# Where VectorE sums a step's bonus: after the previous step's mask, or between the next step's scale and this step's mask

## What is computed

```python
for t in range(S):
    kt, vt, rt = (k[:, :, t], v[:, :, t], r[:, :, t])
    cur = np.einsum('bhd,bhe->bhde', u[None] * kt, vt)
    y[:, :, t] = np.einsum('bhd,bhde->bhe', rt, state + cur)
    state = w[None, :, :, None] * state + np.einsum('bhd,bhe->bhde', kt, vt)
```

## Time and profile before

| | |
|---|---|
| median of 3 runs | 385.12 us (384.98 to 385.4) |
| the profiled execution | 385.27 us |
| its span, first to last instruction | 383.5 us |
| mean granted TensorE clock | 1.000 of full speed |
| PE busy | 369.9 us, 96% |
| DVE busy | 235.0 us, 61% |
| ACT busy | 189.4 us, 49% |
| POOL busy | 94.5 us, 25% |

### The profile page before, as it was taken

How to read it: one execution, slowest core, us unless ns; L and a number is a source line. 1 busy time by engine, 2 the same in 40 slices (tenths; PEclk the granted TensorE clock), 3 DMA queues, 4 the chain that set the end, 5 groups by cost and what they waited for, 6 DMA issues and landing times.

```text
span 383.5 us, 9099 instructions
## 1 busy us (share of the span) xinstructions
PE 369.9 (96%) x3206; PEld 290.6 (76%) x3206; DVE 235.0 (61%) x433; ACT 189.4 (49%) x409; POOL 94.5 (25%) x110
## 2 busy tenths in 40 slices
PE   5698999999999999999999999999999999999996
PEld 5677788878777344577888888888888888888885
DVE  6978787878774301587756556555555555555550
ACT  1344554545434440676564456445644564465452
POOL 4678788878682020100000000000000000000000
PEclk9999999999999999999999999999999999999999
DMA  7899999999999999600011002000200020002002
GB/s 234 286 333 344 400 393 405 399 393 354 405 327 409 390 414 413 249 0 2 1 46 38 0 0 84 0 0 0 82 0 0 0 82 0 0 0 82 0 2 82
DMA packets 21797, 63.76 MB, mean 166 GB/s; under 512 B 3088, under 2 KB 6816, under 8 KB 21392
## 3 DMA queue, kind: packets, MB, share of 16 engines
q1 hardware_dynamic: 20864, 63.09, 43.4%
q10 hardware_dynamic: 912, 0.39, 0.5%
HBM read 58.75 MB, written 4.72 MB: 165 GB/s over the span
## 4 chain that ended last, share of the span: by engine, by line
PE 92%; DVE 2%; DMA 2%; issue 1%; ACT 1%; POOL 1%; SPq 0%; DVEq 0%; ACTq 0%
PE bank L638 11%; PE bank L637 11%; PE bank L636 11%; PE bank L378 6%; PE pair L426 6%; PE pair L636 6%; PE pair L637 6%; PE pair L638 6%; PE bank L623 4%; PE pair L414 3%; PE pair L397 3%; PE bank L585 3%; PE bank L447 3%; PE bank L565 2%; DMA vb<-v 2%; PE bank L438 2%
## 5 line engine op out<-in xcount | busy, mean ns | idle before, releaser
L926 DVE TENSOR_TENSOR gf<-bank,sg 128x512 f32<-128x512 f32 x72 | 49.8, 691 | 58.3 <-ACT sg L1133 58.0
L1133 ACT ACTIVATE sg<-bank 128x512 f32<-128x512 f32 x72 | 42.9, 598 | 71.0 <-PE bank L623 71.0
L637 PE MATMUL bank<-ghi,whi 128*128 128x512 f32 x190 | 73.9, 389 | 0.0
L636 PE MATMUL bank<-glo,whi 128*128 128x512 f32 x190 | 73.9, 389 | 0.0
L638 PE MATMUL bank<-ghi,wlo 128*128 128x512 f32 x190 | 73.9, 389 | 0.0
L937 DVE TENSOR_TENSOR glo<-gf,ghi 128x512 fp32r<-128x512 f32 x96 | 66.3, 691 | 0.3
L1139 ACT ACTIVATE ghi<-gf 128x512 fp32r<-128x512 f32 x95 | 59.3, 624 | 1.8 <-DVE gf L926 1.7
L636 PEld LDWEIGHTS bank<-glo,whi 128*128 128x128 f32 x190 | 35.7, 188 | 7.4
L637 PEld LDWEIGHTS bank<-ghi,whi 128*128 128x128 f32 x190 | 35.7, 188 | 7.4
L638 PEld LDWEIGHTS bank<-ghi,wlo 128*128 128x128 f32 x190 | 35.7, 188 | 7.4
L772 DVE TENSOR_TENSOR rks<-rkb,bank 112x512 f32<-112x512 f32 x48 | 30.8, 681 | 15.4 <-PE pair L414 10.9
(11 more groups left out here) (179 smaller groups left out, 512.3 us busy)
## 6 DMA issues: line engine op xcount, KB each, us to landing
ring<-w SPq DMA_DIRECT2D x24, 512.0 KB, 6.3
rkb<-rk SPq DMA_DIRECT2D x23, 512.0 KB, 6.2
krb<-kr SPq DMA_DIRECT2D x24, 384.0 KB, 5.5
ring<-w SPq DMA_DIRECT2D x4, 1536.0 KB, 14.3
ring<-w SPq DMA_DIRECT2D x8, 768.0 KB, 8.4
vb<-v SPq DMA_DIRECT2D x24, 192.0 KB, 5.5
out<-ob SPq DMA_DIRECT2D x18, 256.0 KB, 2.1
ring<-win SPq DMA_DIRECT2D x3, 1024.0 KB, 14.3
```

What stands on the lines that cost most here:

```text
L636: pe.matmul(o, w_hi, lo, start=(f == 0), stop=False)
L637: pe.matmul(o, w_hi, hi, start=False, stop=False)
L926: dve.tensor_tensor(gf[:, f % 2, :], bank[f % 4][:, :], sg[:, f % 2, :], ALU.mult).then_inc(gf_ok, 1)
L1133: act.activation(sg[:, f % 2, :], bank[f % 4][:, :], ACT.Sigmoid, scale=1.702).then_inc(sg_ok, 1)
```

## The change

In chunks 1 to 5, `bonus_sum` of step n moves on VectorE from the end of step n-1 (behind the mask of n-1) to step n, between the scale of n+1 and the mask of n. In chunk 0 it stays where it was, except that step (0, 3) no longer sums the bonus of (1, 0). No instruction is added or taken away, on any engine; all other lists keep their order.

```diff
                 else:
                     if more:
                         scale(*following(c, b))
+                    if tail:
+                        bonus_sum(c, b)
                     mask(c, b)
                 if is_last(c) and b == 2:
                     row_sum(*early)
-                if more:
+                if is_first(c) and b < B - 1:
                     bonus_sum(*following(c, b))
                 if tail and b == 3:
                     running(c - 1)
```

## The result

| | before | changed |
|---|---|---|
| median of 6 runs | 385.24 us | 396.11 us (395.07 to 397.98) |
| profiled execution, its span | 385.27, 383.5 us | 396.33, 394.6 us |
| mean granted TensorE clock of the profiled execution | 1.000 | 1.000 |

The ratio is 1.0285 with a 95% interval of 1.0248 to 1.0322. I had forecast 390.6 us in 389.0 to 393.8: the sign was right, the size half of what came. In what follows a ratio leaves out executions more than 1.5% above the fastest of their kernel (one each of `e1`, `e2` and `e3`), while a trace is of one execution and can be of such a one.

What follows compares the result with a forecast made beforehand. The prediction took TensorE, running its list without a gap, as the bound. Its terms, 0.53 + 0.48 + 2.2 + 0.29 + 1.91 = 5.4 us, took 385.27 to 390.7; less 0.15, it forecast 390.6 us, range 389.0 to 393.8.

Steps and rivals of the forecast that it cites:

- step (1, 0), with (1, 1): Chain ends 1.73 us late at (1, 0); overlapping the 1.20 us stall soon behind it leaves 0.53 us.
- b = 2 of chunks 1 to 4, b = 3 of chunks 1 to 4: Plain steps: the new chain ends 0.06 us late in each; 0 with a free handover.
- b = 0 of chunks 2 to 4: VectorE comes late to the scale, so TensorE waits about 0.7 to 0.8 us in each; together 2.2 us.
- step (5, 0): Scale and `bonus_turns` are 2.51 us apart, so the chain costs 0.29 us.
- steps (5, 1) to (5, 3): GpSimd's lead is spent; `vd` of (5, 3) comes 1.9 us late, all smaller delays inside it.
- the moved chain: Inside one step: scale, sum, GpSimd's product, then `bonus_turns` on TensorE; 2.80 us from the start of the scale.
- the mask at nothing: The mask moves 0.45 to 0.55 us later but costs nothing in plain steps; in chunk 5 it is inside 1.9 us.
- rival 1: krb and rkb loads come late, each of four chunks losing 0.5 to 1 us more: 392.7 to 394.7; chance 15%.
- Mostly a shorter queue: Argument against late loads: transfers queue behind each other in these chunks, so later issue mostly means a shorter queue.
- VectorE does the same work in the same time: One reduction per step moves, 20 in all, with VectorE's work and time unchanged; only the date of `dds` changes.
- The code stall: TensorE's 1.20 us stand in (1, 1), read as code arriving, overlaps the new wait; the unswallowed rival: 391.8, chance 22%.

Runs made afterwards that it cites:

- e1: The changed kernel with each next-step rkb load issued ahead of this step's krb load; ratio to before 1.0223, about 394.1 us.
- e2: The changed kernel with L831 and L838 rewritten to have one SBUF tensor input each; ratio to before 1.0215, about 393.8 us.
- e3: The changed kernel with the edits of both e1 and e2; ratio to before 1.0200.
- e10: The changed kernel with the load order of e12 and the one-SBUF-input edits of e2; ratio to before 1.0107, 389.7 us.
- e12: The changed kernel with the next step's rkb load issued ahead of the w1 pieces, still behind krb and vb; ratio to before 1.0166, median 392.3 us.
- e11: The kernel before with an added same-size reduction of constants between scale and mask in chunks 1 to 5, sums still early; ratio to before 1.0001.
- e7: The kernel before with only the sums of steps (5, 1) to (5, 3) made late; ratio to before 1.0054, 2.1 us.
- e8: The kernel before with each krb load from chunk 1 on also waiting for the mask's first half two steps earlier; ratio to before 1.0468, 402.4 us.

## Why the prediction was half of what came

| term | predicted | measured | what it was |
|---|---|---|---|
| step (1, 0), with (1, 1) | 0.53 | -0.25 | 1.03 and -1.28 |
| b = 2 of chunks 1 to 4 | 0.24 | 0.0 | as costed, the handover shorter |
| b = 0 of chunks 2 to 4 | 2.2 | 3.2 | 1.9 the chain, 1.3 the long L838 |
| b = 1 of chunks 2 to 4 | none | 1.0 | the long L831 |
| b = 3 of chunks 1 to 4 | 0.24 | 4.0 | rkb late |
| step (5, 0) | 0.29 | 0.8 | 0.35 the chain, 0.4 the long L838 |
| steps (5, 1) to (5, 3) | 1.91 | 2.1 | as costed |
| sum | 5.4 | 10.9 | |

"Measured" is the difference of the two step tables. The 1.3, 0.4 and 1.0 are three times 0.40 to 0.45, 0.42, and three times 0.33 from e10 against e12; the 1.3 counts (2, 0) as its neighbours.

**What held.** The bound, the moved chain and its length (2.80 against 2.71 and 2.86), the place of the waits, the mask at nothing (e11 from (2, 2) on; in the changed kernel TensorE never waits for a mask behind chunk 0), chunk 5's list through GpSimd (1.9 against 2.0 in e7 and 2.1 in the changed kernel), and the cost of about 0.6 in a b = 0 step. Without the two causes below, the terms come to 4.1 us (-0.25 + 1.9 + 0.35 + 2.1) where I had 5.4. Most of this difference lies in step (1, 0), whose loss was 1.03 us and not 1.73: its scale, waiting for rkb, started at 27.99 and not at 28.56. The rest lies in the plain steps, since GpSimd's handover to TensorE took 0.06 us (88.05 to 88.11) instead of 0.14.

**The first step that failed** is the working of rival 1: "by my count it then lands about 0.6 us before GpSimd is free for it, and rkb 1 us before its scale". The prediction doesn't show that count; in it I had SyncE issue rkb soon after krb. The trace shows 2.81 us between the two in SyncE's b = 3 list (75.78 to 78.59), where two w1 pieces go out. A load that lands after a median of 6.6 us (40 to 112 us) and is wanted 5.9 us after its issue (84.50 - 78.59) is late. The trace before had held all of this, for the same two loads:

```profile
69.08 0.33 SPq L277 DMA_DIRECT2D krb<-kr  x1
...
71.91 0.34 SPq L269 DMA_DIRECT2D rkb<-rk  x1
```

The distance was 2.83 us there too, and rkb went out 7.64 us ahead of its scale at 79.55. With the prediction's own 2.2 us taken off, 5.4 are left, less than the median of 6.2 that an rkb load took to land there. That estimate makes it 0.8 us late in each b = 3 step, near the 1.0 that came. "Mostly a shorter queue" was wrong too: the rkb landing took a median of 6.4 us, 6.2 before, so a later issue was a later landing. The queue was short of work at times (347 GB/s over 40 to 112 us, against 383 before). I gave this rival 15% and 1 us a chunk; it was true in size.

**The second step that failed** is "VectorE does the same work in the same time". Its busy time was 235.0 us before and 237.7 after. The change shifted GpSimd's list against VectorE's, and two operations fell on top of GpSimd's. The trace before held the hint: the median of L838 was 0.41 and its shortest 0.21, L831 0.31 and 0.16. The Trainium skill, "SBUF — State Buffer", Who interferes with whom, has the rule: a VectorE instruction with two SBUF inputs takes the read port that GpSimd also reads through, whichever starts first keeps it for its whole instruction, and a VectorE instruction with one SBUF input, outside the modes that use both ports, doesn't contend. With that rule this case's trace agrees, with L831 0.90 us long and ending 0.01 us behind GpSimd's, and e2 with one SBUF input at 0.21. By an estimate from the rule and L1218's 1.00 us, the cost could have been bounded at 1 us for each of the two in a chunk.

**The code stall.** In the changed kernel the 1.20 us of the earlier trace rows are gone: step (1, 1) took 4.57 us for 5.85. But in e7 and e11, where no wait of TensorE stands ahead of it, the same step took 4.56 and 4.24 without a stall, and in e8, where the lists of TensorE and VectorE are those of before, 5.85. So I can't say that the wait swallowed it, and the low total of steps (1, 0) and (1, 1) is no merit of the prediction. Why some of these programs stall there and others don't stays open.

Also open is whether the w1 pieces delay rkb by the time of their issue or by their bytes; e12 moves both.

## What to carry to other kernels

An operation whose result is used a step later is a lead; spend it and follow all that the consumer engine releases, above all the loads behind its buffers, through the issuing queue's own list with the real distance between issues (here 2.8 us for four loads), not only to the engine that waits first. When two engines shift against each other, look for operations of VectorE with two SBUF inputs whose length varies in the trace: here their spread was a wait for GpSimd, and it moved with the shift. A list of loads fits the order in which it is used: the list that served the late sums best cost the early ones 3 us.

## What was not expected of the hardware

TensorE's granted clock, 1.000 in both profiled executions, fell in some others. This is the trace of e1, in slices of 6 us (busy time of PE, PEld, DVE, ACT, POOL, then the clock, DMA share and GB/s):

```profile
66.00:72.00 6.00, 6.00 (x116) 5.25 (x113) 5.03 (x11) 2.88 (x10) 2.01 (x3) 1.00 1.02 392
72.00:78.00 6.00, 3.55 (x48) 2.50 (x42) 2.03 (x4) 0.93 (x2) 5.67 (x7) 0.71 0.93 343
78.00:84.00 6.00, 6.00 (x70) 5.27 (x67) 3.74 (x8) 2.30 (x9) 3.09 (x5) 0.50 0.55 191
84.00:90.00 6.00, 6.00 (x90) 4.82 (x88) 3.41 (x7) 2.54 (x8) 2.86 (x4) 0.93 0.80 302
```

It went from 2.4 to 1.2 GHz in a stretch where TensorE had stood for 2.45 of 6 us, and stayed there for 6 us of full work; steps (3, 0) and (3, 1) took 9.0 and 7.3 us, 6.2 and 4.6 in the changed kernel's own trace. So waits in this stage can cost more than their length. In the six runs of the changed kernel the mean clock was 0.987 to 1.000. It may explain part of the spread of the variants, which wasn't followed, and nothing of the 10.8 us, which were read at a clock of 1.000.
